# Reordering the first loads and the first score of a two-head-at-a-time attention prologue

## What is computed

```python
q_bits = (q @ proj > 0); k_bits = (k @ proj > 0)          # 6 bits each
mask   = bucket(q_bits)[:, None] == bucket(k_bits)[None, :]
scores = where(mask, scale * q @ k.T, -1e9)
attn   = softmax(scores);  x = attn @ v                    # 768 x 64 a head
x = x.reshape(1536, 512)
x = (h - tanh(h)) @ w_out, h = x @ w_in                    # d_ff 2048
out = sum_e p_e * (relu(x @ w1[e]) @ w2[e])                # 4 experts, d_ff 1024
```

## Time and profile before

| | us |
|---|---|
| median of 3 runs (lowest to highest) | 993.88 (993.75 to 993.96) |
| the profiled execution, its own time | 994.03 |
| its span, first to last instruction | 992.2 |
| TensorE busy / VectorE / ScalarE / GpSimd in the span | 983.9 / 674.0 / 462.3 / 443.2 |

### The profile page before, as it was taken

One profiled execution on the slowest core, in us unless ns is written; L12 is line 12 of the kernel. 1 busy time (PEld: TensorE's weight loads), 2 busy tenths in 40 slices (PEclk: granted clock), 3 DMA queues, 4 the chain that ended last, 5 costly groups with the idle time before them and its releaser, 6 DMA issues.

```text
span 992.2 us, 16483 instructions
## 1 busy us (share of the span) xinstructions
PE 983.9 (99%) x5410; PEld 910.3 (92%) x5410; DVE 674.0 (68%) x1127; ACT 462.3 (47%) x852; POOL 443.2 (45%) x436
## 2 busy tenths in 40 slices
PE   8999999999999999999999999999999999999998
PEld 6999999999999999999999888988989899888987
DVE  7888888888856465565996556565565655656555
ACT  6888888888444443444542323223232232322321
POOL 5578779997674463644534304123041230412100
PEclk9999999999999999999999999999999999999999
DMA  5576666652101001010020100201002010020002
GB/s 146 162 185 170 168 167 166 175 163 66 37 22 44 22 24 61 21 42 21 22 64 22 43 22 21 63 21 43 21 21 63 21 42 21 21 64 21 21 18 109
DMA packets 50933, 65.22 MB, mean 66 GB/s; under 512 B 5360, under 2 KB 32720, under 8 KB 50896
## 3 DMA queue, kind: packets, MB, share of 16 engines
q1 hardware_dynamic: 50592, 64.48, 22.8%
q10 hardware_dynamic: 240, 0.30, 0.1%
q0 software_dynamic: 64, 0.00, 0.0%
HBM read 43.87 MB, written 3.19 MB: 47 GB/s over the span
## 4 chain that ended last, share of the span: by engine, by line
PE 94%; DVE 3%; ACT 1%; issue 1%; POOL 0%; DMA 0%; DVEq 0%; ACTq 0%; POOLq 0%
PE ps L1638 34%; PE ps L1661 27%; PE ps L1669 13%; PE ps L1585 7%; PE ps L1555 6%; PE ps L1566 6%; PE ps L1522 2%; DVE hb L1297 1%; DVE pT_lo L1123 0%; DMA proj_raw<-in_proj 0%; POOL g_lo L704 0%; DVE prob L1116 0%; DVE xq_lo L1167 0%; DVE xq_raw L1155 0%; ACT prob L795 0%
## 5 line engine op out<-in xcount | busy, mean ns | idle before, releaser
L1638 PE MATMUL ps<-xq_hi,wu_lo 128*128 128x384 f32 x672 | 227.0, 338 | 1.0 <-ACT hb L912 0.5
L1638 PE MATMUL ps<-xq_hi,wu_hi 128*128 128x384 f32 x672 | 226.2, 337 | 0.0
L1638 PE MATMUL ps<-xq_lo,wu_hi 128*128 128x384 f32 x672 | 226.1, 336 | 0.0
L1328 DVE SCALAR_TENSOR_TENSOR acc<-ps,p_norm,acc 128x512 f32<-128x512 f32 x179 | 134.1, 749 | 100.0 <-PE ps L1661 94.5
L635 POOL TENSOR_TENSOR wu_lo<-wu_raw,wu_hi 128x768 fp32r<-128x768 f32 (+1 forms) x46 | 99.0, 2173 | 222.5 <-ACT wu_hi L839 222.5
L1661 PE MATMUL ps<-wd_lo,g_hi 128*128 128x512 f32 x382 | 150.2, 393 | 0.0
L1661 PE MATMUL ps<-wd_hi,g_hi 128*128 128x512 f32 x382 | 150.1, 393 | 0.0
L1661 PE MATMUL ps<-wd_hi,g_lo 128*128 128x512 f32 x382 | 149.8, 392 | 0.0
L1638 PEld LDWEIGHTS ps<-xq_hi,wu_lo 128*128 128x128 f32 x672 | 126.1, 188 | 6.6 <-issue 1.1
L1638 PEld LDWEIGHTS ps<-xq_lo,wu_hi 128*128 128x128 f32 x672 | 126.2, 188 | 3.9
L1638 PEld LDWEIGHTS ps<-xq_hi,wu_hi 128*128 128x128 f32 x672 | 126.1, 188 | 0.0
(11 more groups left out here) (139 smaller groups left out, 1764.1 us busy)
## 6 DMA issues: line engine op xcount, KB each, us to landing
wu_raw<-in_w SPq DMA_DIRECT2D x64, 128.0 KB, 2.8
wd_raw<-in_w SPq DMA_DIRECT2D x16, 512.0 KB, 3.4
q_raw<-in_qT SPq DMA_DIRECT2D x28, 192.0 KB, 3.2
k_raw<-in_kT SPq DMA_DIRECT2D x28, 192.0 KB, 3.3
wu_raw<-in_w_in SPq DMA_DIRECT2D x32, 128.0 KB, 2.5
wd_raw<-in_w_out SPq DMA_DIRECT2D x8, 512.0 KB, 3.5
v_raw<-in_vP SPq DMA_DIRECT2D x16, 192.0 KB, 2.8
inv_rows<-inv_dram SPq DMA_DIRECT2D x16, 192.0 KB, 3.2
```

The costliest lines, as they stand in the source:

```text
L1328: dve.scalar_tensor_tensor(out=part_of, in0=source, scalar=scale, in1=part_of, op0=ALU.mult, op1=ALU.add).then_inc(down_taken, 1)
L1638: mm = pe.matmul(to, w[:, wslot, k, :], x[:, xslot, k, :], start=start and k + m == 0, stop=k == 1 and m == 2, skip_group_check=not start)
```

## The change

The first query half, the projection and the first transfer of the keys' second half each become the first of a queue of their own. The keys' half 0 becomes the second of the ScalarE queue (lane 0) and of the SyncE queue (lane 1). The projection is one transfer that reads the 64x6 matrix twice (a leading dimension of two with no stride) and writes 128 partitions, in place of two transfers of 64. VectorE makes the projection's parts before the rest of the first query half. The first score (query tile 0 of head 0) makes its pair (`q_hi`, `k_st`) first, and waits for the bits only ahead of the pair (`q_lo`, `k_hi`).

```diff
@@ SyncE
-                for n in range(2):
-                    load_first(sp, q_raw, qT[0], q0_loaded, n)
-                load_first(sp, k_raw, kT[0], k0_loaded, 1)
+                load_first(sp, q_raw, qT[0], q0_loaded, 0)
+                load_first(sp, k_raw, kT[0], k0_loaded, 0, 1)
+                load_first(sp, q_raw, qT[0], q0_loaded, 1)
                 load_halves(sp, q_raw_of(1), head_of(qT, 1), q_loaded)
@@ GpSimd
-                load_halves(pool, proj_raw, proj, p_loaded)
+                for lane in range(2):
+                    load_first(pool, k_raw, kT[0], k0_loaded, 1, lane)
                 pool.memset(proj_f32[:], 0.0).then_inc(const_ready, 1)
@@ ScalarE
-                for lane in range(2):
-                    load_first(act, k_raw, kT[0], k0_loaded, 0, lane)
-                load_first(act, k_raw, kT[0], k0_loaded, 1, 1)
+                act.dma_start(proj_raw[:], proj.unsqueeze(0).broadcast_to([2, D, BITS])).then_inc(p_loaded, 16)
+                load_first(act, k_raw, kT[0], k0_loaded, 0)
                 for n in range(2):
                     first_round(n)
@@ VectorE
-                first_q_rest(0)
-                dve.wait_ge(p_loaded, 32)
+                dve.wait_ge(p_loaded, 16)
                 dve.wait_ge(const_ready, 1)
...
+                first_q_rest(0)
                 first_k_rest(0)
                 first_q_rest(1)
                 first_k_rest(1)
@@ TensorE, score
-                    if qt == 0:
+                    if qt == 0 and not at_zero(h):
                         pe.wait_ge(bits_taken, h + 1)
                         wait(pe, spread_ready, 48 * h)
-                        if at_zero(h):
-                            pe.wait_ge(k_hi0_ready, 1)
-                            pe.wait_ge(k0_bits_first, 1)
-                            pe.wait_ge(q0_bits_first, 1)
...
                     parts = ((q_lo[b], k_hi[b]), (q_hi[b], k_st[b]))
+                    if at_zero(h) and qt == 0:
+                        parts = parts[::-1]
                     for m, (x, y) in enumerate(parts):
+                        if at_zero(h) and qt == 0 and m == 1:
+                            pe.wait_ge(k_hi0_ready, 1)
+                            pe.wait_ge(bits_taken, 1)
+                            pe.wait_ge(k0_bits_first, 1)
+                            pe.wait_ge(q0_bits_first, 1)
```

## The result

The changed kernel is slower: 995.06 us median (994.69 to 995.61, 22 runs), against 993.82 (993.39 to 994.32, 22 runs) before; the slowest run of the kernel before lies below the fastest of the changed one. The ratio is 1.0013, with a 95% interval of 1.0007 to 1.0019, so 0.7 to 1.9 us. The profiled execution took 995.22, its span is 993.3.

The account below looks back on a forecast made before the run. TensorE, at 94% of the span, bounds the kernel; only the start can move. The first clamp gains 0.59 (chain) and 0.35 (score), less 0.1, so 0.84: 993.19 for the profiled execution, 993.0 median, range 992.7 to 994.3.

Parts of the forecast that it names:

- Key half 0: First key loads, second on ScalarE's and SyncE's queues: landing taken as 5.24 again, bounds 4.0 to some 5.9.
- the sum: At the first clamp, 10.65 instead of 11.59: 0.59 from the chain, 0.35 from the score, 0.1 taken back; 0.84 gained.
- VectorE's four rests: On VectorE after the projection parts: four rests in place of three, 4 x 0.58 = 2.32, first bit step at P + 3.71.
- the 0.65 of a bit step: VectorE's bit steps: the key step of half 1 ends one step (0.65) before the last, at 9.95.
- the score's 0.35: First score on TensorE: only the pair with bits left, 0.61 in place of 0.98; 0.35 of the clamp's gain.
- The projection: First on ScalarE's queue, issued at 0.75 in place of 2.04: to land between 3.35 and 4.2.
- Rival 2: ScalarE's first transfer: projection split over two engines lands slowly, kernel slower, 993.9 to 998.4; chance 0.16.
- P: Landing time of the projection: above 4.3 it starts to cost, above 5.15 the kernel is slower than before.
- the signs of being wrong: In the profile after: VectorE idle on the projection past 4.3, key rounding after 5.3, query half 1 awaited after 6.0, others.
- Does it carry?: Head 1's preparation: GpSimd's key rest ends at 14.56, TensorE asks at 14.82; holds with 0.26 to spare, later rows move along.
- the meeting of three paths near 8.0: Before the first bit step: VectorE, ScalarE and warm-up paths meet near 8.0, so none has to be right to 0.1.
- the 0.94: First clamp at 10.65 instead of 11.59: 0.94 earlier, 0.59 from the chain and 0.35 from the score.

Follow-up runs that it names:

- two transfers: Changed kernel with the projection as two transfers of 64 rows at the head of ScalarE's queue, keys' lane 0 behind both; median 993.52 us.
- 128 partitions outermost: Changed kernel, first transfer on ScalarE's queue reading 128 rows of 24 bytes from the expert probabilities in place of the projection twice; median 993.34 us.
- the mended kernels: Changed kernel with the projection as two 64-row transfers: both heading ScalarE's queue (993.52 us), or one there behind the keys, one first on GpSimd's (993.59).
- the kernel with the strided source: Changed kernel, first transfer on ScalarE's queue reading 2 x 64 rows of expert probabilities, leading dimension strided in place of zero; single run 994.72 us.

## Why the prediction was wrong

Forecast were 993.0 and a range up to 994.3; it came to 995.06. By its own steps:

- *Key half 0* is the step that failed: "I take 5.24 again: same place in the queue, same bytes asked for before it." It was 6.96, past even the bound of 5.9. (The 5.24 was lane 1's, second on that queue; lane 0 had been its first.) The place in a queue was counted, and not the time that the transfer ahead takes to issue: the prediction gave ScalarE's two issues "some 0.6 less" than the three of before, and they took until 2.66 where three had taken until 2.60. The 1.36 are a property of the form that no row of before had. The second transfer of the queue went out at 2.14, some 0.8 later than the second of before, and took 4.8 to land in place of 3.9: together the 1.72. The 0.9 is head 1's traffic, which the later issue met: with that held back it took 3.8, no more than before.
- Put the measured 6.96 into the sum and the rest holds: 10.65 + 1.72 = 12.37, measured 12.43. VectorE's four rests, the 0.65 of a bit step and the score's pair were right; the score's 0.35 at the clamp measured 0.33.
- *The projection* landed at 3.29, just below the range of 3.35 to 4.2. In the second place of the queue it took 4.76.
- *Rival 2* had the transfer, the queue and the two engines right, and the sign. It was priced at the wrong place: the small writes cost 9 ns each, not 13.5 to 30, and P, 3.29, never came near 5.15. The loss came through what stands behind the transfer in its queue, for which the rival allowed 0.7. That 995.06 lies within its 993.9 to 998.4 is luck: its mechanism for P did not occur. Of the signs of being wrong, the key rounding after 5.3 came, the idle VectorE past 4.3 for the projection did not. Its chance, 0.16, was too low for a rule that named this very form.
- *Does it carry?* The loss does: 0.84 at the clamp, 0.92 at the first weighing, 1.09 at the end. Of the gains not every one did, between the profiled executions: against the kernel before, the clamp 0.54 early (two transfers) took 0.6 off the span, 1.07 early (128 partitions outermost) 0.7, 0.86 early (the score's part alone) 0.1.
- *The gain that was to be had* was overstated too. Of the kernels with the changed loads only one, at 10.52, had its first clamp as early as the 10.65 forecast; the mended kernels had 11.05 and 11.12, held up by the warm-up (7.68) and by the projection (4.65). The prediction took the meeting of three paths near 8.0 as a comfort, but the latest of the three sets the pace, and each moved by some 0.5 or more between executions. The medians are 0.15 to 0.42 below the kernel before, not 0.84, and none of these differences clears its interval. The profiled execution of before (994.03) had later landings than the one with the score's part alone, which has the same loads, so part of the 0.94 was that execution's bad luck. How much is open.
- *What can be told.* The prediction put at 2 us what a measurement can tell from no change. With 22 runs of each kernel 1.24 was told: the interval of 0.7 to 1.9 leaves no change out.

## What to carry to other kernels

Before a small transfer is put at the head of a queue, ask how many engines its outermost dimension lets it use. On ScalarE's queue two 64-row transfers took less to issue (1.21) than one transfer of 2 x 64 (1.36), and what stands behind it in the queue pays. Cost a queue by the issue time and the form of each transfer, not by places and bytes. And where one execution is the base of a forecast of less than a microsecond, compare its landings with a second one first.

## What the runs showed that was not expected

- Issue on ScalarE's queue for 128 rows of 24 bytes: 0.40 from a 128-row source, 0.67 as 16 x 8, and 1.36 as 4 x 32 or 2 x 64.
- A late issue is amplified: out at 1.98 the keys' lane 0 landed at 5.4, out at 2.14 behind the two-way transfer at 6.96. It is not that the small writes ahead of it end later: those of the two-way transfer were over by 3.2 us, those of the second 64-row transfer ran on past it (80 packets of that queue from 2.8 to 3.6 us). Head 1's traffic, 0.52 behind the keys in the changed kernel and 0.94 behind them with two transfers, accounts for 1.0; what the other 0.4 (3.8 against 3.4) comes from was not settled, and 0.3 of it can be chance, since the same loads with four warm-up matmuls took 3.7.
- With the same five warm-up matmuls, TensorE was free between 6.96 and 7.81, here in the kernel with the strided source. In the kernel before, their starts are 0.64 apart up to 5.34 and 0.32 from 5.83 on, while the granted clock reads 1.00 throughout; when that turn comes differs from execution to execution:

```profile
4.70 3.11 PE L1624 MATMUL ps<-x_f 128*128 128x384 f32 x5
```

- In the kernel without the score's part TensorE's granted clock was at 0.50, the lower level of 1.2 GHz, from 13 to 15 us, after it had stood idle from 11.1 to 11.99 and for other stretches before. In the changed kernel, whose first score fills part of that hole, it stayed at 1.00. With one profile of each, that the filled hole keeps the clock up is a guess, and the kernel before speaks against it as the whole story: TensorE stood idle there from 9.67 to 10.59 ahead of the same four matmuls, and its clock stayed at 1.00.
